# The second layer of a dense mixture of experts by one level of Strassen's algorithm

## The reference

```
h = np.maximum(x @ w1[e], 0.0)     # 2304 x 1024
ye = h @ w2[e]                     # 2304 x 512
out += P[:, e:e + 1] * ye
```

## Time and profile before

| | |
|---|---|
| median of 3 runs | 1113.91 us |
| profiled execution | 1115.35 us, with a span of 1113.6 us |
| PE busy | 1080.4 us (97%), 5815 matmuls |
| PEld busy | 861.3 us (77%), 5815 weight loads |
| DVE busy | 465.0 us (42%) |
| ACT busy | 327.2 us (29%) |
| POOL busy | 145.5 us (13%) |
| mean granted TensorE clock | 0.971 |

### The profile page before, as it was taken

The page is one execution under the profiler, slowest core; times in us unless marked ns, Lnnn a source line. Parts: engine busy times, 40 slices in busy tenths (PEclk is TensorE's granted clock), DMA queues, the critical chain, the costliest instruction groups (busy, mean ns, idle before and its releaser), DMA issues.

```text
span 1113.6 us, 15960 instructions
## 1 busy us (share of the span) xinstructions
PE 1080.4 (97%) x5815; PEld 861.3 (77%) x5815; DVE 465.0 (42%) x1179; ACT 327.2 (29%) x882; POOL 145.5 (13%) x218
## 2 busy tenths in 40 slices
PE   7999968799999999999999999999999999999998
PEld 5888832178888888888888888888888888888887
DVE  6766642045754243433343343334333443343331
ACT  6777612042223222321232132213221322131120
POOL 6545410012000200110021002100210021000000
PEclk9999979569999999999999999999999999999999
DMA  5773199922020202020202020202020200000111
GB/s 180 260 265 115 39 361 383 351 76 69 8 77 1 75 2 76 1 76 1 76 3 76 1 76 1 76 1 77 2 76 1 76 1 1 0 1 29 48 48 48
DMA packets 36849, 87.17 MB, mean 78 GB/s; under 512 B 2976, under 2 KB 2976, under 8 KB 36768
## 3 DMA queue, kind: packets, MB, share of 16 engines
q1 hardware_dynamic: 36768, 86.07, 21.6%
HBM read 81.35 MB, written 4.72 MB: 77 GB/s over the span
## 4 chain that ended last, share of the span: by engine, by line
PE 94%; DMA 3%; DVE 1%; ACT 1%; issue 0%; POOL 0%; SPq 0%; POOLq 0%; DVEq 0%
PE bank L681 24%; PE bank L682 24%; PE bank L683 24%; PE bank L640 6%; PE bank L482 3%; PE bank L492 3%; PE bank L511 3%; PE bank L592 2%; PE bank L624 2%; DMA slot_raw<-slot_w_in 1%; PE bank L529 1%; DMA early_raw<-slot_w_in 1%; DMA q_ring<-q_tiles 1%; PE bank L567 1%; PE bank L523 1%; PE bank L661 0%
## 5 line engine op out<-in xcount | busy, mean ns | idle before, releaser
L681 PE MATMUL bank<-w_hi,h_hi 128*128 128x512 f32 x1152 | 452.4, 393 | 0.0
L682 PE MATMUL bank<-w_lo,h_hi 128*128 128x512 f32 x1152 | 450.9, 391 | 0.0
L683 PE MATMUL bank<-w_hi,h_lo 128*128 128x512 f32 x1152 | 448.8, 390 | 0.0
L767 ACT ACTIVATE h_hi<-bank 128x384 fp32r<-128x384 f32 x384 | 157.5, 497 | 593.0 <-PE bank L640 593.0
L967 DVE SCALAR_TENSOR_TENSOR h_lo<-bank,h_hi 128x384 fp32r<-128x384 f32 x384 | 187.4, 551 | 191.9 <-ACT h_hi L767 191.6
L683 PEld LDWEIGHTS bank<-w_hi,h_lo 128*128 128x128 f32 x1152 | 216.7, 188 | 46.9
L681 PEld LDWEIGHTS bank<-w_hi,h_hi 128*128 128x128 f32 x1152 | 216.6, 188 | 45.9 <-issue 3.1
L682 PEld LDWEIGHTS bank<-w_lo,h_hi 128*128 128x128 f32 x1152 | 216.6, 188 | 40.9
L1017 DVE SCALAR_TENSOR_TENSOR acc<-bank,gate_now,acc 128x512 f32<-128x512 f32 x126 | 94.5, 750 | 299.2 <-PE bank L683 299.2
L456 POOL TENSOR_TENSOR w_lo<-w_raw,w_hi 128x512 fp32r<-128x512 f32 x56 | 71.3, 1289 | 705.4 <-ACT w_hi L746 705.4
L640 PE MATMUL bank<-c_stack,g_stack 128*128 128x384 f32 x384 | 85.4, 344 | 0.1
(11 more groups left out here) (126 smaller groups left out, 445.5 us busy)
## 6 DMA issues: line engine op xcount, KB each, us to landing
w_raw<-big_w_in SPq DMA_DIRECT2D x16, 2048.0 KB, 8.3
slot_raw<-slot_w_in SPq DMA_DIRECT2D x18, 1024.0 KB, 9.3
early_raw<-slot_w_in SPq DMA_DIRECT2D x8, 1024.0 KB, 13.7
q_ring<-q_tiles SPq DMA_DIRECT2D x18, 256.0 KB, 4.3
k_ring<-k_tiles SPq DMA_DIRECT2D x18, 256.0 KB, 4.8
v_ring<-v_rows SPq DMA_DIRECT2D x18, 256.0 KB, 2.7
out_rows<-acc SPq DMA_DIRECT2D x18, 256.0 KB, 2.0
late_raw<-slot_w_in SPq DMA_DIRECT2D x4, 1024.0 KB, 12.7
```

Source lines behind the costliest of these rows:

```text
L681: pe.matmul(to, h_hi[b][:, f, col], w2_hi[parity][:, f, :], start=(f == 0), stop=False)
L682: pe.matmul(to, h_hi[b][:, f, col], w2_lo[parity][:, f, :], start=False, stop=False)
L683: done = pe.matmul(to, h_lo[b][:, f, col], w2_hi[parity][:, f, :], start=False, stop=(f == FT - 1))
L767: act.activation(h_hi[c % 2][:, f, :], bank[H_BANK[n % H_BANKS]][:, 0:CT], ACT.Relu).then_inc(h_hi_ready, 1)
```

## The change

The second layer of the second mixture is computed in Winograd's form of Strassen's algorithm, one level. A is the relu output of a pair of token tiles, B is w2[e]. A's rows are the two tiles of the pair, its columns the two halves of the inner 1024; B's rows are the same halves and its columns the two halves of the output's 512. Eight products of 128 x 512 by 512 x 256 become seven, for which four sums of blocks of A (S1 to S4) and four of B (T1 to T4) are made. The seven stand in the order A11, A12, S1, S2, A22, S4, S3 against B11, B21, T1, T2, T4, B22, T3. Three of them (S2, S4, S3) go on in the bank that VectorE has already read, so that some of the output sums form in PSUM.

- TensorE: a product is 4 blocks x 3 matmuls of 256 columns; 9 pairs x 7 products an expert. Products go round three banks (`bank_of`) and wait for the add of the product three before. `hidden` makes 128x256 blocks, two to a bank, four banks; for the next pair it comes ahead of products 0 and 2.
- ScalarE: `relu_halves` rounds relu of A11 and of the second tile's and second half's blocks, and keeps plain copies; `sum_hi` rounds the four sums; `weight_hi` rounds the seven sides of B, two in pair 5 and five in the last pair of an expert.
- VectorE: `sums_first` and `sums_second` make the sums and the rests of the unsummed blocks; `add_product` adds each product to its target in `acc` (product S3 to both halves); `weight_lo` for T1 and B22.
- GpSimd: the rests of the four sums of a pair (`sum_lo`), the sums of B and five rests of B's sides.
- The gate steps of the first expert stand ahead of the adds of products in `ROUND_AT`; the first 14 tiles are added unscaled, and ScalarE scales them in the last two pairs.
- One buffer `raw` takes w1 and w2 of later experts in turn. `t_split`, B's sides, lies where the RAW ring was. So parts from 16 on reuse the early, extra and late buffers alone (`AGAIN` is 9 instead of 12), and the first w2 is loaded after part 18.

The core of the diff:

```diff
-    AGAIN = BUFFERS - LATE_RAW
+    AGAIN = BUFFERS - RAW_RING
-        return n if n < BUFFERS else (n - BUFFERS) % AGAIN
+        return n if n < BUFFERS else RAW_RING + (n - BUFFERS) % AGAIN
-    W2_FIRST_AFTER = 3 * PARTS // 4 - 3
+    W2_FIRST_AFTER = BUFFERS + 2
+    TP = TILES // 2
+    HF, HD2 = FT // 2, D // 2
+    PRODUCTS = 7
+    PER_EXPERT = PRODUCTS * TP
+    A11, A12, S1, S2, A22, S4, S3 = range(PRODUCTS)
+    B11, B21, T1, T2, T4, B22, T3 = range(PRODUCTS)
+    FRESH = (A11, A12, S1, A22)
+    ROUND_AT = [(2, 0), (2, 4), (3, 2), (4, 0), (4, 4), (5, 2), (6, 0), (6, 4)]
+    UNSCALED = ROUND_AT[-1][0] + 1
...
# TensorE
+            def product(e, p, k, parity, first):
+                n, slot = TP * e + p, (parity + p) % 2
+                if not first or PRODUCTS * p + k >= 3:
+                    pe.wait_ge(added, PRODUCTS * n + k - 2)
...
+                if first:
+                    gate_step(p, k)
+                if p == 0:
+                    if k in (T1, B22):
+                        pe.wait_ge(t_lo_vec_ready, 2 * e + (T1, B22).index(k) + 1)
+                    else:
+                        pe.wait_ge(t_lo_ready, 5 * e + (B11, B21, T2, T4, T3).index(k) + 1)
...
+                to = bank[bank_of(p, k)][:, 0:HD2]
+                for f in range(HF):
+                    pe.matmul(to, left[:, 0, f, :], t_place(parity, k, 0)[:, f, :], start=(f == 0 and k in FRESH), stop=False,
+                              skip_group_check=k not in FRESH)
+                    pe.matmul(to, left[:, 0, f, :], t_place(parity, k, 1)[:, f, :], start=False, stop=False,
+                              skip_group_check=k not in FRESH)
+                    last = pe.matmul(to, left[:, 1, f, :], t_place(parity, k, 0)[:, f, :], start=False, stop=(f == HF - 1),
+                                     skip_group_check=k not in FRESH)
+                last.then_inc(product_ready, 1)
...
+                for p in range(TP):
+                    ahead = not (last and p == TP - 1)
+                    e1, p1, parity1, n1, before = next_pair(e, p, parity, first)
+                    for k in range(PRODUCTS):
+                        if ahead and k == 0:
+                            hidden(e1, p1, parity1, 0, n1, before)
+                        if ahead and k == 2:
+                            hidden(e1, p1, parity1, 1, n1, before)
+                        if not last and (p, k) == (G_TILE_PAIR, 3):
+                            pe.wait_ge(g_lo_ready, GROUPS * e + GROUPS)
+                            g_products(e + 1)
+                        product(e, p, k, parity, first)
...
# ScalarE
+                    for s in range(2):
+                        relu_halves(n1, (parity1 + p1) % 2, s, before)
...
+                    sum_hi(n1, 0, before)
+                    if crunch:
+                        weight_hi(e + 1, parity1, T1, w2_rows)
+                    sum_hi(n1, 1, before)
+                    if crunch:
+                        weight_hi(e + 1, parity1, T2, w2_rows)
+                        weight_hi(e + 1, parity1, T4, w2_rows)
+                    sum_hi(n1, 2, before)
+                    if crunch:
+                        weight_hi(e + 1, parity1, B22, w2_rows)
+                    sum_hi(n1, 3, before)
+                    if crunch:
+                        weight_hi(e + 1, parity1, T3, w2_rows)
...
+                    if first and p >= UNSCALED:
+                        act.wait_ge(gate_vec, 5 + SINKHORN_ROUNDS)
+                        for t in range(UNSCALED * (p - UNSCALED), UNSCALED * (p - UNSCALED + 1)):
+                            act.wait_ge(added, PRODUCTS * (t // 2 + 1))
+                            act.activation(acc[:, t, :], acc[:, t, :], ACT.Copy, scale=gates[:, t, 0:1]).then_inc(acc_scaled, 1)
...
# VectorE
+                    for k in range(PRODUCTS):
+                        add_product(e, p, k, first)
+                        if ahead and k in (0, 2):
+                            sums_first(n1, (parity1 + p1) % 2, k // 2, before)
+                        if ahead and k in (1, 3):
+                            sums_second(n1, (parity1 + p1) % 2, k // 2, before)
+                        if not first and (p, k) == (0, 0):
+                            weight_lo(e, parity, B22, w2_rows, t_lo_vec_ready)
+                        if not last and (p, k) == (TP - 1, 5):
+                            weight_lo(e + 1, 1 - parity, T1, w2_rows, t_lo_vec_ready)
+                        if not last and k == 4 and STACK_TILE_PAIR <= p < STACK_TILE_PAIR + GROUPS:
+                            g_lo(e + 1, 1 - parity, p - STACK_TILE_PAIR)
```

More of the change, by code:

```diff
@@ L217, in attention_then_two_moes @@
[L217 to L223, removed]
-            ("h_hi1", [P, FT, CT], F32R), ("h_lo1", [P, FT, CT], F32R))
@@ L626, in g_products, with hidden @@
                 last.then_inc(g_ready, 1)
-            g_products(0, first=True)
+            def hidden(e, p, parity, s, n, before):
+                for b, f, quarter in ((4 + 2 * s, HF + 2 * s, 2 * s), (3 + 2 * s, 2 * s, 2 * s + 1)):
+                    if p == 0:
+                        pe.wait_ge(g_lo_ready, GROUPS * e + quarter + 1)
+                    if before:
+                        if b % 2:
+                            pe.wait_ge(a11_lo_ready, 2 * n + s - 1)
+                        else:
+                            pe.wait_ge(a2_lo_ready, 2 * n + s - 1)
+                            pe.wait_ge(s_sum_ready, 8 * n + 4 * s - 4)
+                    for j in range(2):
+                        last = pe.matmul(bank[b][:, j * 2 * P:(j + 1) * 2 * P], g_stack[parity][:, (f + j) * P:(f + j + 1) * P],
+                                         c_stack[:, 2 * p * P:2 * (p + 1) * P], start=True, stop=True)
+                    last.then_inc(h_ready, 1)
@@ L955, in _, with g_lo @@
-            g_lo(0)
+            def g_lo(e, parity, i):
+                q = QUARTER_ORDER[i]
+                dve.wait_ge(g_hi_ready, GROUPS * e + i + 1)
+                cols = slice(q * QUARTER, (q + 1) * QUARTER)
+                stack = g_stack[parity]
+                exact, rounded = bank[7][q * SLOTS:(q + 1) * SLOTS, 0:QUARTER], stack[q * SLOTS:(q + 1) * SLOTS, cols]
+                for to in (4 - q, q) if q % 2 else (1, 3):
+                    last = dve.tensor_tensor(stack[to * SLOTS:(to + 1) * SLOTS, cols], exact, rounded.bitcast(F32), ALU.subtract)
+                last.then_inc(g_lo_ready, 1)
@@ new lines, in expert @@
+                for p in range(TP):
+                    ahead = not (last and p == TP - 1)
+                    _, p1, parity1, n1, before = next_pair(e, p, parity, first)
+                    for k in range(PRODUCTS):
[10 more added lines that the diff above has]
+                            g_lo(e + 1, 1 - parity, p - STACK_TILE_PAIR)
```

516 lines of the change are left out of this document (299 added, 217 removed).

## The result

The changed kernel takes 1143.07 us, the median of 4 runs (1141.38 to 1143.59), beside 1113.96 us (1113.61 to 1114.49) for the kernel before: ratio 1.026, 95% interval 1.024 to 1.028. It is slower by 2.6%, where 1.3% faster was forecast, and 1 us outside the range. The profiled execution took 1143.59 us with a span of 1141.8.

What follows compares the result with a forecast made beforehand. TensorE was taken as the bound (94% of the span). Start 243.5 + matmuls 804.5 + 13.3 + gate 3 + cold clock 2 + expert 0 extra 2 + stalls 28 + tail 3.2 = 1099.5 span, forecast 1100 us, range 1052 to 1142.

Steps and rivals of the forecast that it cites:

- expert 0: Sinkhorn rounds on VectorE ahead of adds, and g split work, stall pairs 2 to 6 by 11 us in all.
- Where the cover is gone: Stalls in the second MoE: rounds in the first expert 11 us, its end 9.3, six other expert changes 7.5.
- Sum of stalls 28: TensorE's waits across the second MoE's eight experts total 28 us, bounds 0 and 60.
- Rival D: Sums passing VectorE, ScalarE, GpSimd wait at each step; stalls 60 instead of 28 us, total 1132; chance 13%.
- the pace: Second-layer 256-column matmuls, each with its own weight load: 120 ns, 121.6 with contention; 6616 take 804.5 us.
- 13.4 ns: Time per matmul beyond streaming, taken as fixed from 512 columns (227 less 213.3); with 106.7 streaming gives 120 ns.
- 2% of contention: Matmuls slow from 227 to 231 ns while ScalarE and VectorE split hidden blocks; counted two thirds of the time, 1.3%.
- Rival B: Each matmul's time beyond streaming shrinks with columns: 113.5 ns, 115 with contention, 44 us less, 1056; chance 15%.
- Rival C: The weight load no longer hides under each of 6616 matmuls: 128 ns, 42 us more, 1142; chance 22%.
- the start: Before the first product: slot-weight part 16 issues at 172.2 instead of 163.00, delaying everything 6.5 us; first product at 243.5.
- the first change of experts: End of the first expert: ScalarE's scaling of acc and weight splits delay relus; TensorE loses 2.9 + 6.4 = 9.3 us.
- the other changes: Six later expert changes: weight splits end 2.8 us into the next pair, product 6 starts 1.25 late; 7.5 us.

Runs made afterwards that it cites:

- `g_hi` early: Kernel after, with ScalarE copying its quarter of the next expert's g stack right behind the relus instead of behind the sums' roundings: 1101.71 us, ratio 0.989.
- written out: Kernel after with the early g stack copy and all eight experts in code without a loop: 1102.43 us, ratio 0.990.

## Why the prediction was wrong

The span was forecast at 1099.5 and measured at 1141.8. By terms, + where the kernel took longer:

| term | difference, us | from |
|---|---|---|
| wait at the g split, seven experts | +41 | `g_hi` early: 41.4 less |
| expert 0 beyond that | +5 | 126.4 against 123.5, at a faster pace |
| the seven expert changes | +7.5 | first pairs of 11 with `g_hi` early |
| loop's jump, 2 x 2.0 | +4 | written out |
| first product, 244.44 for 243.5 | +0.9 | stretches |
| plain pair 10.88 to 11.04 for 11.19 | -16 | stretches |
| sum | +42.4 | measured +42.3 |

The terms are rounded, and that they meet to 0.1 us is luck: a microsecond more for the seven G products (2.05 each, forecast 1.9) is in none of them. With the first four, the stalls forecast at 28 were about 85, beyond their bound of 60 and outside the 15 to 42 named as a sign of being wrong. The expert changes and the jump aren't independent, as told above.

**The step that failed** is "Where the cover is gone", with its "Sum of stalls 28". The g split entered it as "0.9 more from pair 4 on for the g split (two of 0.42)", work on VectorE, in expert 0 only. As work it was sized rightly (0.86). It was a wait that the change made: `g_lo` went from a place between tiles to a place inside a pair, while `g_hi` went behind a step that needs the pair's last product. Asking, for the one instruction, "what is the last thing before its releaser on the releaser's engine, and what does that wait for", gives it from the code and rows at hand: `sum_hi` S3 can't start before product 6 ends, add 4 is done some one and a half products (2.2 us) earlier, and 0.65 for `sum_hi` and 0.8 for two of `g_hi` (0.39 each in the earlier trace rows) follow: 3.65 us. I asked what stands *behind* the waiting adds and never what stands *ahead* of the split's releaser.

**Rival D** ("slower: handovers", 13%) had the kind but not the place: it saw a loss in the handovers of any pair, and the plain pairs lose nothing. The loss sits in 28 pairs of 72, about 1.5 us each.

**Right: the pace.** TensorE's timeline of the kernel after, 23 steps from the first of these rows to the last, 2.76 us:

```profile
620.04 0.28 PE L768 MATMUL bank<-t_split,s_split 128*128 128x256 f32 x1
...
622.80 0.28 PE L772 MATMUL bank<-t_split,a 128*128 128x256 f32 x1
```

120.0 ns each, the "13.4 ns" of rest fixed and the weight load hidden. The 2% of contention was not there: the plain pair has 120 with VectorE busy for 72% of it. Rival B (113.5, "the rest shrinks") is not what happens at the forecast's place of the buffers; the 113 to 117 of the shifted buffers show that the rest is no constant of the engine either, but my B gave the reason wrongly. Rival C (128) is out; that its 1142 lies 1 us from the measured time is chance, since no step was near 128.

**Right: the start**, the slot-weight part issued late (172.43 for 172.2) and +7.5 for +6.5. The last figure is good to some 3 us only: in the kernels here that share this opening, the first product comes at 241.3 to 246.8. Two rows of the kernel after, where the earlier trace rows have the issue at 163.00 and the last part's matmuls at 217.19:

```profile
172.43 2.09 SPq L396 DMA_DIRECT2D early_raw<-slot_w_in  x3
...
225.19 1.93 PE L671 MATMUL bank<-late_raw,hid_wide 128*32 128x512 f32 x8 [0.65 <-DMA late_raw<-slot_w_in]
```

**Right in size, by luck in part: the first change of experts**, ScalarE's scaling ahead of the relus. ScalarE, VectorE and TensorE of the kernel after:

```profile
381.39 4.38 ACT L942 ACTIVATE acc<-acc,gates 128x512 f32<-128x512 f32 x7
...
386.11 0.18 DVE L1231 COPY gate_now<-gates 128x18 f32 x1 [6.34 <-ACT acc L942]
...
387.20 0.58 PE L768 MATMUL bank<-t_split,s_split 128*128 128x256 f32 x1 [4.49 <-DVE acc L1220]
```

The first pair of expert 1 lost 7.0 us against the 6.4 forecast. But the wait is 4.5 of it; behind it 18 matmuls run at the lower granted level (0.50, 1.2 GHz), 213 ns instead of 120, which is 1.7 more and was no term. And spreading the scaling took off only 1.8, so it was a smaller part than the forecast made it.

**Too small: expert 0.** The rounds stop TensorE in the pairs named, but VectorE's operations with both inputs in SBUF grow beside GpSimd, and the clock answers. VectorE in a round of expert 0, the TensorE wait behind it, the stretch of the pair that follows, and its first 5.1 us alone:

```profile
314.17 1.33 DVE L1183 TENSOR_TENSOR gates<-gates,gate_stat 128x144 f32<-128x144 f32 x1
...
317.00 0.31 DVE L1160 TENSOR_TENSOR gates<-gates,row_stat 128x144 f32<-128x144 f32 x1
...
318.13 0.58 PE L768 MATMUL bank<-t_split,a 128*128 128x256 f32 x1 [3.64 <-DVE acc L1214]
...
318.30:332.70 14.40, 14.24 (x97) 13.94 (x98) 10.35 (x30) 3.87 (x9) 2.90 (x3) 0.82 0.01 2
318.30:323.40 5.10, 5.10 (x24) 5.10 (x25) 3.36 (x8) 0.00 (x0) 0.00 (x0) 0.50 0.00 0
```

Two operations of one size, 1.33 and 0.31: GpSimd works until 316.62, so beside the first and not beside the second. Behind the wait of 3.64 the pair runs at a mean granted clock of 0.82. Its first 24 matmuls stand at 0.50 (1.2 GHz) and take 5.3 us, 213 ns a step, where 2.9 would do at 1.00: 2.4 of the 3.5 us that the pair takes over the plain pair's 10.88. So a wait of 3.64 costs 6. In expert 0 the clock was 0.92 against 0.98 before, and 2 us were forecast for it. The sum itself had a slip: by its own 13.7 against 11.2, pair 2 loses 2.5, not 3.1.

**Too small: the other changes**, forecast 1.25 us each. With `g_hi` early the first pairs of experts 2 to 7 lose 3.6, 0.7, 3.6, 0.6, 2.3 and 3.6. I took VectorE's weight rest at 1.2 and it is up to 3.3 beside GpSimd. The loop's jump was no term at all: in the kernel before TensorE has no idle time at it.

Open stays which relation of addresses sets the rest of a matmul (the moving operand was shifted, in two kernels, and in the second two buffers of weights with it), how expert 0's loss divides into rounds, shared port and clock, and why its clock differs from run to run, with which four of these kernels spread over 4 to 9 us.

## What to carry to other kernels

A change that moves an instruction which another engine waits for is priced by its wait, not by its duration: for each such pair, look at what stands just ahead of the releaser on its own engine and what that needs, and then at what stands behind the waiter. If a change of this size disappoints, compare a stretch where it works alone (10.88 us for a plain pair) with one where it doesn't before judging the idea: here moving two lines turned 2.6% slower into 1.1% faster, and with 64 bytes of offset into 2.4%. Durations of VectorE operations with both inputs in SBUF (1.22 or up to 3.3 us here) hold only for the GpSimd load at which they were read.

## What the runs showed of the hardware

- The start-to-start step of a 256-column float32r matmul with its own 128x128 weight load was 120 ns with the moving operand at a multiple of 512 bytes or 256 below it, 119 on average at 128 below (one run), 114 to 117 at 64 below; for 512 columns a shift of 64 bytes made a mean of 227.9 into 229.2.
- Each loop jump left TensorE idle for 1.5 to 1.9 us at steps of 120 ns, and none at steps of 227 ns.
- Behind a wait of 3.6 us TensorE ran 24 matmuls at a granted clock of 0.50, at 213 ns instead of 120.
- A VectorE operation of 128x1024 with both inputs in SBUF took 1.22 us, and up to 3.3 beside GpSimd; one of 128x256 with an input in PSUM took 0.48 in both.
